# Two-layer MLP after attention on one core: in the first tile of the second layer, low parts of the weights made by VectorE in pieces, weight sums paced, GpSimd sums held back

## The reference

```python
def _moe_ref(x, w_in, w_out, s, b):          # first layer
    h = x @ w_in
    r = np.maximum(h, 0.0)
    g = s * (r * r) + b
    return g @ w_out

def _moe2_ref(x, w_in, w_out):               # second layer
    h = x @ w_in
    g = h - np.tanh(h)
    return g @ w_out

def reference(**kwargs):
    attn_out = _attn_ref(q, k, v)            # 4 x 8 heads x 576 x 64: pooled attention + a band of 7 keys
    x = attn_out.transpose(0, 2, 1, 3).reshape(2304, 512)
    x = _moe_ref(x, w_in, w_out, s, b)       # 512 -> 2048 -> 512
    return _moe2_ref(x, w_in2, w_out2)       # 512 -> 2048 -> 512
```

## Time and profile before

| | us |
|---|---|
| median of 3 runs | 908.61 |
| lowest, highest | 908.51, 908.93 |
| profiled execution, its time | 906.39 |
| its span | 904.2 |
| mean granted clock of PE | 0.994 |

### The profile page before, as it was taken

How to read it: one execution, slowest core, us unless ns; L and a number is a source line. 1 busy time by engine, 2 the same in 40 slices (tenths; PEclk the granted TensorE clock), 3 DMA queues, 4 the chain that set the end, 5 groups by cost and what they waited for, 6 DMA issues and landing times.

```text
span 904.2 us, 15887 instructions
## 1 busy us (share of the span) xinstructions
PE 879.7 (97%) x5956; PEld 823.2 (91%) x5956; DVE 586.6 (65%) x759; ACT 471.9 (52%) x1128; POOL 416.3 (46%) x372
## 2 busy tenths in 40 slices
PE   7999999999999999999999878999999999999998
PEld 6889999999999999999999767989889888989887
DVE  5658599989999999982201587454844447543444
ACT  3899585467546755445656434334543336433332
POOL 6568474966497653525726653213431125212110
PEclk9999999999999999999999989999999999999999
DMA  8972453353344123102103321101420101401012
GB/s 216 276 240 55 126 145 85 89 128 86 97 114 104 58 59 80 35 2 96 36 28 94 110 92 32 39 24 47 140 70 24 47 24 26 115 24 47 24 47 71
DMA packets 57903, 73.56 MB, mean 81 GB/s; under 512 B 19110, under 2 KB 36068, under 8 KB 57828
## 3 DMA queue, kind: packets, MB, share of 16 engines
q1 hardware_dynamic: 56233, 72.12, 28.8%
q10 hardware_dynamic: 1595, 0.43, 0.2%
HBM read 63.10 MB, written 9.44 MB: 80 GB/s over the span
## 4 chain that ended last, share of the span: by engine, by line
PE 92%; DVE 4%; ACT 2%; issue 1%; DMA 1%; SPq 1%; ACTq 0%; DVEq 0%
PE acc L2197 23%; PE hid L2169 22%; PE hid L2234 19%; PE acc L2251 14%; PE pa L2251 7%; PE pa L2127 1%; PE pa L2094 1%; DMA dkey<-in_k_dram 1%; PE pa L1969 1%; PE pa L2111 1%; DVE sum L1628 1%; PE pa L2140 1%; DVE wq_raw L1576 1%; DVE g2l L1633 0%; PE acc L1961 0%
## 5 line engine op out<-in xcount | busy, mean ns | idle before, releaser
L1233 POOL TENSOR_TENSOR gl<-relu,gh 128x288 fp32r<-128x288 f32 x128 | 129.5, 1016 | 155.2 <-PE acc L2197 109.8
L1249 POOL TENSOR_TENSOR w2bl<-w2b_raw,w2bh 128x512 fp32r<-128x512 f32 x48 | 62.4, 1320 | 213.4 <-ACT w2bh L1890 213.4
L2197 PE MATMUL acc<-gh,wbh 128*128 128x288 f32 (+1 forms) x512 | 154.5, 302 | 0.0
L2169 PE MATMUL hid<-xh,wah 128*128 128x288 f32 x512 | 153.5, 301 | 0.3 <-ACT relu L1859 0.2
L2197 PE MATMUL acc<-gl,wbh 128*128 128x288 f32 (+1 forms) x512 | 151.5, 296 | 0.0
L2197 PE MATMUL acc<-gh,wbl 128*128 128x288 f32 (+1 forms) x512 | 151.2, 295 | 0.0
L2169 PE MATMUL hid<-xh,wal 128*128 128x288 f32 x512 | 150.4, 295 | 0.0
L2169 PE MATMUL hid<-xl,wah 128*128 128x288 f32 x484 | 142.0, 294 | 0.0
L2234 PE MATMUL hid<-x2h,wqh 128*128 128x384 f32 x336 | 113.4, 337 | 11.5 <-DVE sum L1613 4.9
L1859 ACT ACTIVATE relu<-hid 128x288 f32<-128x288 f32 x128 | 52.3, 408 | 130.6 <-PE hid L2169 109.8
L2234 PE MATMUL hid<-x2l,wqh 128*128 128x384 f32 x336 | 113.5, 338 | 0.0
(11 more groups left out here) (209 smaller groups left out, 1884.6 us busy)
## 6 DMA issues: line engine op xcount, KB each, us to landing
w2b_raw<-in_moe_w_out_dram SPq DMA_DIRECT2D x24, 512.0 KB, 3.7
kl<-in_k_dram SPq DMA_DIRECT2D x23, 240.0 KB
vl<-in_v_dram SPq DMA_DIRECT2D x23, 240.0 KB
x2T<-ystage SPq DMA_DIRECT2D x8, 576.0 KB, 3.2
own<-in_q_dram SPq DMA_DIRECT2D x11, 384.0 KB
wa_raw<-in_moe_w_in_dram SPq DMA_DIRECT2D x4, 1024.0 KB, 8.6
wb_raw<-in_moe_w_out_dram SPq DMA_DIRECT2D x4, 1024.0 KB, 10.2
x2raw<-x2T SPq DMA_DIRECT2D x10, 384.0 KB, 3.9
```

What stands on the lines that cost most here:

```text
L1233: g.tensor_tensor(out=gl[:, turn % LRING1, 0:NS], in0=relu[:, f % 2, :], in1=gh[:, turn % GRING1, 0:NS].bitcast(F32), op=ALU.subtract).the ...
L1249: g.tensor_tensor(out=w2bl[:, slot, :], in0=w2b_raw[:, slot, :], in1=w2bh[:, slot, :].bitcast(F32), op=ALU.subtract).then_inc(s_w2bl, 1)
L2169: one = pe.matmul(dst, w[:, group, d, cols], x[:, j % XRING, d, :], start=i == 0, stop=i == 3 * KT - 1)
L2197: one = pe.matmul(acc[:, d, n], w[:, f, cols], g[:, turn % ring, n], start=(f == 0 and p == 0), stop=(f == FT - 1 and p == 2))
```

## The change

Seven edits, all around tile 0 of layer 2:

- `w2a_high` and `w2a_low` go in three pieces of 3, 2 and 2 of the seven combinations (768, 512, 512 columns), and `w2a_low` moves from GpSimd to VectorE.
- `w2b_low` of steps 0 to 7 moves to VectorE, as two pieces. From step 8 on it stays with GpSimd.
- `w2_sums(q)` follow `u2(q - 2)` in the plan, for q > 1.
- `t1` of tiles 1 and 2 waits at run time for p1 of step 8j - 3.
- PE's order in a step starts with p6. Steps 0, 1 and 23 have orders of their own.
- `finish1` of the last tile goes in four pieces, and `out2(0, i)` waits for its own bank's piece alone.
- Line numbers move: L1573 to L1586 and so on.

```diff
+W2PARTS = [(0, 3), (3, 5), (5, 7)]
+EARLY2 = 3
...
-        o.add("DVE", 1.8, (2, q), ("w2_sums", q), [("load_w2a", q)])
-        o.add("ACT", 1.65, (2, q), ("w2a_high", q), [("w2_sums", q)])
-        o.add("POOL", 4.7, (2, q), ("w2a_low", q), [("w2a_high", q)])
+        paced = [("u2", q - 2)] if q > 1 else []
+        o.add("DVE", 1.8, (2, q), ("w2_sums", q), [("load_w2a", q)] + paced)
+        for part, (m0, m1) in enumerate(W2PARTS):
+            o.add("ACT", 0.2 + 0.22 * (m1 - m0), (2, q), ("w2a_high", q, part), [("w2_sums", q)])
+            o.add("DVE", 0.17 + 0.26 * (m1 - m0), (2, q), ("w2a_low", q, part), [("w2a_high", q, part)])
...
         o.add("ACT", 1.25, (2, n), ("w2b_high", n), [("load_w2b", n)])
-        o.add("POOL", 2.9, (2, n), ("w2b_low", n), [("w2b_high", n)])
+        if n < QUADS:
+            for f in range(2):
+                o.add("DVE", 0.7, (2, n), ("w2b_low", n, f), [("w2b_high", n)])
+        else:
+            o.add("POOL", 2.9, (2, n), ("w2b_low", n), [("w2b_high", n)])
...
+            if j:
+                before.append(("product", QUADS * j - EARLY2, "p1"))
             o.add("POOL", 1.2, (1, j, kk), ("t1", j, kk), [("load_x2", j, kk)] + before)
...
-        order = ["p1", outs[0], "p6", outs[1], "p2", "p7", outs[2], "p4", outs[3], "p5", outs[4], "p3", outs[5]]
+        order = (["p6", "p1", outs[0], "p2", "p7", outs[1], "p4", "p5", outs[2], "p3"] if n == 0 else
+                 ["p6", "p1", outs[0], outs[1], "p2", outs[2], "p7", outs[3], "p4", "p5", outs[4], "p3", outs[5]] if n == 1 else
+                 ["p6", outs[0], "p1", outs[1], "p2", "p7", outs[2], "p4", outs[3], "p5", outs[4], "p3", outs[5]])
         if n == TILES2 * QUADS - 1:
+            order = ["p6", "p1", outs[0], outs[1], "p2", "p7", outs[2], "p4", "p5", outs[3], "p3", outs[4], outs[5]]
...
-                    after.append(("w2a_low", q))
+                    after.append(("w2a_low", q, len(W2PARTS) - 1))
...
-                after = [chain, ("w2b_low", one)] + [("g2_low", one, m) for m in ((0, 1) if i < BLOCK2 // 2 else (2, 3))]
+                after = [chain, ("w2b_low", one, 1) if one < QUADS else ("w2b_low", one)] + [("g2_low", one, m) for m in ((0, 1) if i < BLOCK2 // 2 else (2, 3))]
...
-                    after.append(("finish2", one // QUADS - 1, i) if one else ("finish1", last))
+                    after.append(("finish2", one // QUADS - 1, i) if one else ("finish1", last, min(i, KT - 1)))
...
-                    o.add("ACT", 1.9, (0,), ("finish1", last), [chain, ("store1", last - 1)])
-                    o.add("SP", 0.6, (0, last), ("store1", last), [("finish1", last)], kbytes=600)
+                    for d in range(KT):
+                        o.add("ACT", 0.48, (1,) if d else (0,), ("finish1", last, d), [chain, ("store1", last - 1)])
+                    o.add("SP", 0.6, (0, last), ("store1", last), [("finish1", last, KT - 1)], kbytes=600)
...
-            elif kind == "w2a_low":
-                q, = key
-                g.wait_ge(s_w2ah, q + 1)
-                g.tensor_tensor(out=wql[q][:, :, :, :], in0=wq_raw[q][:, :, :, :], in1=wqh[q][:, :, :, :].bitcast(F32),
-                                op=ALU.subtract).then_inc(s_w2al, 1)
-
             elif kind == "w2b_low":
                 n, = key
+                if n == QUADS:
+                    g.wait_ge(s_w2bl, 2 * n)
                 for f in range(2):
...
+                if j:
+                    g.wait_ge(s_product["p1"], QUADS * j - EARLY2 + 1)
...
+            elif kind == "w2a_low":
+                q, part = key
+                mats = slice(*W2PARTS[part])
+                ve.wait_ge(s_w2ah, len(W2PARTS) * q + part + 1)
+                ve.tensor_tensor(wql[q][:, mats, :, :], wq_raw[q][:, mats, :, :], wqh[q][:, mats, :, :].bitcast(F32),
+                                 ALU.subtract).then_inc(s_w2al, 1)
+
+            elif kind == "w2b_low":
+                n, f = key
+                slot = n % 2 * 2 + f
+                ve.wait_ge(s_w2bh, 2 * n + f + 1)
+                ve.tensor_tensor(w2bl[:, slot, :], w2b_raw[:, slot, :], w2bh[:, slot, :].bitcast(F32), ALU.subtract
+                                 ).then_inc(s_w2bl, 1)
...
+                j, *banks = key
                 sc.wait_ge(s_used, FT * (j + 1))
+                banks = banks or range(KT)
...
-                for d in range(KT):
+                for d in banks:
...
-                i, = key
+                i, part = key
+                mats = slice(*W2PARTS[part])
                 sc.wait_ge(s_w2sum, 4 * (i + 1))
-                sc.activation(wqh[i][:, :, :, :], wq_raw[i][:, :, :, :], ACT.Copy).then_inc(s_w2ah, 1)
+                sc.activation(wqh[i][:, mats, :, :], wq_raw[i][:, mats, :, :], ACT.Copy).then_inc(s_w2ah, 1)
...
-                    pe.wait_ge(s_w2al, q + 1)
+                    pe.wait_ge(s_w2al, len(W2PARTS) * (q + 1))
...
-                    pe.wait_ge(s_y, KT * TILES1)
+                    pe.wait_ge(s_y, KT * (TILES1 - 1) + min(i, KT - 1) + 1)
```

More of the change, by code:

```diff
@@ L1867, in scalar_program @@
             elif kind == "finish1":
-                j, = key
+                j, *banks = key
                 sc.wait_ge(s_used, FT * (j + 1))
+                banks = banks or range(KT)
                 if j == 0:
```

## The result

| | before | after |
|---|---|---|
| median (us) | 908.59 (908.51 to 908.93, 4 runs) | 894.98 (894.02 to 895.96, 4 runs) |
| profiled execution: time, span | 906.39, 904.2 | 894.99, 893.1 |
| mean granted clock of PE | 0.994 | 0.996 |
| step 0 to step 3 (S3 - S0) | 59.50 | 43.43 |
| step 0 to step 23 (S23 - S0) | 373.11 | 361.77 |

The ratio is 0.985, 95% interval 0.9833 to 0.9867: 1.5% faster, clear of the scatter of the runs, inside the range, 0.3 from the forecast of 894.7. Two terms behind that number were wrong all the same, and they come first where the trace is read.

A forecast was written before the change was run, and what follows sets the result against it. PE bounds the kernel, kept waiting in steps 0 to 2 by VectorE instructions that GpSimd's low parts hold. 15.9 recoverable less 2.0 in step 5 gives 13.9 off the 908.61 median: 894.7 us, range 891.4 to 899.5.

The forecast's parts named there:

- What can be had back: PE from step 0 to step 3: 59.50 before, 43.6 if packed, so 15.9 us lost in all.
- Rival 3: Long VectorE rows are the price of their operands, not GpSimd's doing: 36 us more, 928; chance 0.03.
- Rival 2: In-order VectorE queue: w2b_low waits for a late transfer in front of u3, steps 2 to 7: +8, 902.7; chance 0.18.
- Order of PE and finish1: Step 0 and out2 of bank 0: pairing sums get cover, zero stall; the tightest place, 1 to 2 us once if it fails.
- Weight sums paced: w2_sums(q) follow u2(q-2); their transfers start two steps ahead, so hidden, no cost.
- GpSimd sums held back: Step 5: t1 and t3 alternate with VectorE's sums, u3 is late for p4, PE loses 2.0 us once.
- rival 1: VectorE is served first in step 5, so no 2.0 us loss: 892.7, down to 891.9; chance 0.22.
- Tile change: T2's chain starts 2.4 later, p6 is due 2.4 earlier: nothing taken, 0.8 us in all each way for the range.
- The sum: 15.9 - 2.0 = 13.9 us gained: span 890.3, profiled execution 892.5, plus 2.2 to the median, 894.7.

The follow-up runs named there:

- e1: The changed kernel with the low parts of weights made by GpSimd again (quads in the same three pieces), all else kept: 901.36 us, ratio to before 0.993.
- e3: The changed kernel with the old order of PE (p1, out, p6, out, p2) in steps 8 and 16 alone: 897.58 us.
- e8: The changed kernel with the old order of PE (p1, out, p6, out, p2) in steps 7 to 22: 893.45 us.
- the probe: Changed kernel without hold, old order in steps 7 to 22, step 7's w2b_low on GpSimd; added GpSimd subtraction, copy, memset in steps 2, 3, 4: 891.01 us.
- e2: The changed kernel with t1 and t3 of a later tile held one step longer, to step 6: 892.91 us.
- e5: The changed kernel without the wait that holds t1 and t3 of tiles 1 and 2 back: 892.86 us.
- e10: The changed kernel without the hold of t1 and t3 and with w2b_low of step 7 on GpSimd, new order of PE kept: 893.89 us.

## Why the prediction was right, and where it wasn't

**The cause and its size: right.** "What can be had back" was 15.9; steps 0 to 2 gave 16.07, at the starts that were forecast (515.5, 531.1, 546.7 against 515.61, 531.27, 546.91), at a granted clock of 1.00, with no VectorE row over 1.3 between 505 and 575. Rival 3 (long rows as the price of the operands) is out: the moved 768 columns take 0.95 and the next instruction follows after 0.90, 512 take 0.68 and 0.60, against estimates of 0.88 and 0.61. Rival 2 (a late transfer in the in-order queue) did not appear: PE waits for nothing in steps 0 to 4. The Trainium skill (VectorE: DVE Perf Modes, section on the TRN2 errata) would give 0.96 and 0.69 for lengths by its formula, and the rows agree with 0.95 and 0.68; spacing is what fills a queue. With such lengths as spacing the stall of step 5 comes to 2.2, where the forecast says 2.4.

The mechanism (GpSimd holds a VectorE instruction with two SBUF inputs, the pairing sum behind it is late, PE waits) is shown in rows of before, after, e1, e3 and e8, by the probe with nothing else on GpSimd, and from both sides: taking GpSimd's low parts away gains 12.1 by itself, putting them back costs 6.4. That the move alone gave the 15.9 back is not shown: of the 16.07 of steps 0 to 2 the move alone had 11.9 (47.59 against 59.50), and the other edits without it 14.1 (45.43), which they then paid for with 5.4 in steps 3 to 5. Either cure does most of it there; only both together keep steps 0 to 4 all at 15.66 or less. Each edit also passes through `plan()`, which may put other work in another place, and no run moves the low parts with every other order fixed.

**"Order of PE and finish1": right, and worth 4.2 together.** The moved low parts alone left 4.2 more in steps 0 and 1, with PE waiting for pairing sums and never for `finish1`; without the hold or without the pacing these steps are as in the change. I had named the place the tightest and costed it at zero, which it was.

**"Weight sums paced" and "GpSimd sums held back": right in kind, 0.4 too dear.** I had forecast 2.0 in front of p4 of step 5 and 1.57 came. What failed is the count of sums between the GpSimd rows: I took t1 and t3 as a pair with a sum only behind it, so that two sums were left over; in fact a sum fitted behind each row, the fourth ended at S5 + 8.62, and `u3` at S5 + 9.7 where I had 10.3 (my terms add up to 10.2). That settles rival 1 too: VectorE isn't served first, they take turns. What I had not seen is that the cost needs the pacing too; without it the hold is free.

**"Tile change": wrong.** "Nothing taken, 0.8 in all each way" was 3.1 (1.41 and 1.72). I had looked at the products' operands, T2's chain, and found it in time, which it was: its second low part ended 9.5 after step 7's start (620.51), where I had 10. The late one was another: `copy1`, behind a `g2_high` on ScalarE that hangs on a held `dif`, and behind two `x2_high`, with one output as cover where three pieces of PE work had stood. The mechanism is the one of the forecast (GpSimd holds VectorE), at a place where GpSimd's low parts of x were left; I had checked the edit there for what it makes late, and not for what cover it takes from the waits that exist. The runs bear this out from both sides: the old order from step 7 on mends steps 15 and 16, and with `w2b_low` of step 7 on GpSimd again, steps 7 and 8 too.

**The sum: right by two errors that cancel.** By its terms the span was to be 890.3; it was 893.1: 3.1 more at the tile changes, 0.4 less in step 5, 0.3 of later start, 0.2 less in steps 0 to 2. The step from the profiled execution to the median, 2.2, was to be added again; after the change it was 0.0 (894.99 against 894.98). The time around the span was 1.9, not 2.2. So 2.8 too low, 2.2 and 0.3 too high: that the forecast came within 0.3 of the median is luck. The second profile of the kernel before shows why it should not have been: step 2 alone varied by 0.6 there, at a granted clock of 0.90 or 1.00 behind PE's idle times, and those idle times are what the change removed.

## What to carry to other kernels

If GpSimd and VectorE both work on SBUF operands, look at GpSimd's busy time in the windows where a cheap VectorE instruction is long; moving the work to VectorE cost 3.3 us of VectorE's queue per step and won 12 by itself. Leaving it on GpSimd, but in pieces, paced and behind another order of products, won 6.6; the two do not add up. Around such a move, an order of products is worth its cover at one place and may cost it at the next: test it by step, since here the new order (with the pieces of `finish1`) won 4.2 in steps 0 and 1, and together with the moved `w2b_low` of step 7 it lost 3.1 at the tile changes. And a hold or a pacing put in together with the real cure should be taken out once on its own; of the two here neither gained beside the other and the pair cost 1.6.

## What the runs showed that I had not expected

- When both wait, GpSimd and VectorE take turns, instruction by instruction, in all rows looked at (583.07 to 586.8 above): the length of GpSimd's instruction, not its share, sets how long each VectorE one lasts. A held row ends 0.27 to 0.29 behind GpSimd's, in step 5 after and beside the subtraction alike. GpSimd is held as well: in e2 its t3 (598.59) took 1.46 beside a `w2bl` of VectorE that had begun at 598.49, where it takes 1.01 with VectorE idle (502.38 in e5).
- A mended wait can uncover a longer one in a step before: e3 lost 2.6 where 2.1 was to be gained, and in e10 the 0.53 that went from one wait came back as 0.45 in the next.
- In two executions of the kernel before, PE's idle times of steps 0 to 2 add up nearly alike but lie differently, and the granted clock of step 2 was 1.00 in one and 0.90 in the other, 0.6 of 16.7.
